# Mixing weights that travel with the token numbers, and a new order for the last two experts' loads

## The reference

```python
# 1: attention inside 16 clusters (q, k, v: 2 x 8 x 768 x 64); x has shape (1536, 512)
# 2: mixture of 8 experts, each takes exactly cap = N // 8 = 192 tokens
order = np.argsort(-(x @ w_gate).flatten())
for idx in order:
    tok, e = (int(idx) // E, int(idx) % E)
    if assigned[tok] >= 0 or counts[e] >= cap:
        continue
    assigned[tok] = e
    counts[e] += 1
for e in range(E):
    mask = assigned == e
    out[mask] = np.maximum(x[mask] @ w1[e], 0.0) @ w2[e]
# 3: 4 dense experts, mixed by given weights
p = domain_probs / (domain_probs.sum(-1, keepdims=True) + 1e-09)
for e in range(4):
    out += p[:, e:e + 1] * (np.maximum(x @ v1[e], 0.0) @ v2[e])
```

## Time and profile before

| | us |
|---|---|
| median of 3 runs (lowest, highest) | 1040.72 (1040.03, 1041.43) |
| the profiled execution | 1038.46 |
| its span in the trace | 1036.7 |
| PE busy | 1002.0 (97%) |
| DVE, ACT, POOL busy | 605.8, 444.0, 440.9 |

### The profile page before, as it was taken

How to read it: one execution, slowest core, us unless ns; L and a number is a source line. 1 busy time by engine, 2 the same in 40 slices (tenths; PEclk the granted TensorE clock), 3 DMA queues, 4 the chain that set the end, 5 groups by cost and what they waited for, 6 DMA issues and landing times.

```text
span 1036.7 us, 18055 instructions
## 1 busy us (share of the span) xinstructions
PE 1002.0 (97%) x6542; PEld 920.8 (89%) x6542; DVE 605.8 (58%) x1320; ACT 444.0 (43%) x862; POOL 440.9 (43%) x360
## 2 busy tenths in 40 slices
PE   5999999999998999998999999999999999999996
PEld 4889999999987999998998899998899998899995
DVE  4888888888866444444224555544487544455542
ACT  4888888888830111111333233223253323233320
POOL 5042323233101111112575875565557765576542
PEclk9999999999999999999999999999999999999998
DMA  4223232323155967679921221221212421221201
GB/s 113 74 77 85 76 83 80 80 82 78 30 124 116 228 167 153 206 190 239 210 60 63 79 65 62 82 72 51 83 41 82 142 81 43 82 75 50 80 1 62
DMA packets 87745, 99.62 MB, mean 96 GB/s; under 512 B 18560, under 2 KB 57472, under 8 KB 87680
## 3 DMA queue, kind: packets, MB, share of 16 engines
q1 hardware_dynamic: 84976, 92.40, 33.0%
q0 software_dynamic: 2704, 6.33, 2.0%
HBM read 79.81 MB, written 6.32 MB: 83 GB/s over the span
## 4 chain that ended last, share of the span: by engine, by line
PE 92%; DVE 3%; ACT 2%; DMA 1%; POOL 1%; issue 1%; SPq 0%; DVEq 0%; POOLq 0%
PE ps_y L1431 9%; PE ps_y L1432 9%; PE ps_y L1430 9%; PE ps_h L1457 9%; PE ps_y L1472 7%; PE ps_h L1432 6%; PE ps_h L1430 6%; PE ps_h L1431 6%; PE ps_t L1335 6%; PE ps_s L1322 4%; PE ps_s L1323 3%; PE ps_o L1350 3%; PE ps_o L1349 3%; PE ps_m L1296 2%; PE ps_m L1369 2%; PE ps_m L1282 1%
## 5 line engine op out<-in xcount | busy, mean ns | idle before, releaser
L577 POOL TENSOR_TENSOR w_lo<-w_sum,w_hi 128x1792 fp32r<-128x1792 f32 x32 | 129.8, 4078 | 62.4 <-ACT w_hi L795 62.4
L1432 PE MATMUL ps_y<-b_lo,h_hi 128*128 128x512 f32 x384 | 149.7, 390 | 0.0
L1431 PE MATMUL ps_y<-b_hi,h_lo 128*128 128x512 f32 x384 | 149.7, 390 | 0.0
L1430 PE MATMUL ps_y<-b_hi,h_hi 128*128 128x512 f32 x384 | 149.4, 389 | 0.0
L1249 DVE SCALAR_TENSOR_TENSOR Y<-ps_y,mix_n,Y 128x512 f32<-128x512 f32 x84 | 63.0, 750 | 134.9 <-PE ps_y L1432 134.9
L1430 PE MATMUL ps_h<-x_hi,w_hi 128*128 128x384 f32 x384 | 128.6, 335 | 0.0
L1432 PE MATMUL ps_h<-x_lo,w_hi 128*128 128x384 f32 x384 | 128.5, 335 | 0.0
L1431 PE MATMUL ps_h<-x_hi,w_lo 128*128 128x384 f32 x384 | 128.4, 334 | 0.0
L583 POOL TENSOR_TENSOR b_lo<-b_raw,b_hi 128x2048 fp32r<-128x2048 f32 x16 | 74.0, 4626 | 115.2 <-ACT b_hi L802 115.2
L974 DVE TENSOR_TENSOR p_lo<-ps_t,p_hi 128x384 fp32r<-128x384 f32 x192 | 100.0, 548 | 27.9 <-ACT p_hi L725 26.3
L965 DVE TENSOR_REDUCE neg_max<-ps_s 128x1 f32<-128x768 f32 x96 | 91.3, 951 | 17.9 <-PE ps_s L1323 17.9
(11 more groups left out here) (203 smaller groups left out, 2224.8 us busy)
## 6 DMA issues: line engine op xcount, KB each, us to landing
w_sum<-in_moe_w_dram SPq DMA_DIRECT2D x64, 256.0 KB, 3.2
b_raw<-in_moe_w_dram SPq DMA_DIRECT2D x16, 1024.0 KB, 5.2
raw_a<-in_moe_w_dram SPq DMA_DIRECT2D x8, 1024.0 KB, 8.7
raw_b<-in_moe_w_dram SPq DMA_DIRECT2D x8, 1024.0 KB, 13.0
odd_a<-in_moe_w_dram SPq DMA_DIRECT2D x8, 1024.0 KB, 7.5
odd_b<-in_moe_w_dram SPq DMA_DIRECT2D x8, 1024.0 KB, 14.7
khhT<-kqT SPq DMA_DIRECT2D x32, 192.0 KB, 2.8
raw_k<-in_k_dram SPq DMA_DIRECT2D x16, 192.0 KB, 2.4
```

What stands on the lines that cost most here:

```text
L577: g.tensor_tensor(w_lo[t][:], w_sum[t][:, 1:8], w_hi[t][:].bitcast(F32), ALU.subtract).then_inc(wlo_done[t], 1)
L1430: t_.matmul(dst, w_hi, x_hi, start=first, stop=False)
L1431: t_.matmul(dst, w_lo, x_hi, start=False, stop=False)
L1432: return t_.matmul(dst, w_hi, x_lo, start=False, stop=last)
```

## The change

`place` gets 12 more columns per tile: each of the four mixing weights in three bf16 parts whose sum is the fp32 number (DVE splits them at the start, four more instructions after L1029; `domain_probs` is loaded in the layout of `place`). The one-hot product then has 14 columns instead of 2 and yields token number and weights; a new function `token_mix(n)` adds the three parts (three DVE instructions on 96 x 8 elements) and leaves the four weights behind the token number in `ids`, 5 words per slot. `keep_ids` waits for it and stores 192 pieces of 20 bytes instead of 192 of 4 bytes. One load brings all 1536 slots' 5 words back to `ids_all`; the 12 gathers, the second read of the numbers and the store of `mix_rows` are gone. Stage 3 takes its factors from `ids_all`. In the last part of the search `token_ids(6)` is written ahead of `take_slots(7)`. On SP the w2 loads of expert 6 wait for its row gather as those of the others do, and the w1 loads of expert 7 wait until both halves of w2 of expert 6 have landed.

```diff
@@ SP, expert_weights(n)
                 to_a, to_b = (((raw_a, a_in), (raw_b, b_in)), ((odd_a, odd_a_in), (odd_b, odd_b_in)))[n % 2]
+                if n == E - 1:
+                    sp.wait_ge(b_in[1], 16 * (n // 2 + 1))
                 for i in range(2):
                     at_least(sp, h_full, 8 * (n - 2) + 4 * i + 4)
                     load_a(*to_a, 0, e, i)
                 at_least(sp, y_full, 2 * (n - 2) + 2)
-                if n < E - 2:
+                if n < E - 1:
                     sp.wait_ge(gathered, 32 * (n + 1))
@@ POOL
             def keep_ids(n):
                 first = n * CAP
-                g.dma_start(ids_dram[first:first + CAP].rearrange("(s p) o -> p (s o)", s=2), ids[0:CAP // 2, n, :],
-                            allow_slow_non_contiguous=True).then_inc(ids_out[n >= EARLY], 16)
+                pool.wait_ge(mix_ready, n + 1)
+                g.dma_start(ids_dram[first:first + CAP].rearrange("(s p) o -> p s o", s=2), ids[0:CAP // 2, n],
+                            allow_slow_non_contiguous=True).then_inc(ids_out, 16)
...
-            for n in range(EARLY):
+            for n in range(E):
                 expert_rows(n)
                 keep_ids(n)
-            pool.wait_ge(ids_out[0], 16 * EARLY)
-            ids_by_tile(0, 0, T_EARLY)
...
-            for t in range(T_EARLY, NT):
-                mix_rows(t)
+            pool.wait_ge(ids_out, 16 * E)
+            g.dma_start(ids_all[:], ids_dram.rearrange("(t p) o -> p t o", p=P),
+                        allow_slow_non_contiguous=True).then_inc(ids_back, 16)
@@ DVE, at the start
+            mlink(v_.tensor_copy(place[:, :, 2:2 + E2], mix_n[:]), 5)
+            mlink(v_.tensor_tensor(mix[:], mix_n[:], place[:, :, 2:2 + E2], ALU.subtract), 6)
+            mlink(v_.tensor_copy(place[:, :, 2 + E2:2 + 2 * E2], mix[:]), 7)
+            mlink(v_.tensor_tensor(place[:, :, 2 + 2 * E2:], mix[:], place[:, :, 2 + E2:2 + 2 * E2],
+                                   ALU.subtract), 8)
@@ DVE, search
+            def token_mix(n):
+                HS = CAP // 2
+                at = ps_tok[0:HS, 0:2 * W].rearrange("p (s a) -> p s a", s=2)
+                link(v_.tensor_copy(mix_lo[0:HS], at[:, :, 2 + 2 * E2:]))
+                link(v_.tensor_tensor(mix_mid[0:HS], mix_lo[0:HS], at[:, :, 2 + E2:2 + 2 * E2], ALU.add))
+                v_.tensor_tensor(ids[0:HS, n, :, 1:].bitcast(F32), mix_mid[0:HS], at[:, :, 2:2 + E2],
+                                 ALU.add).then_inc(mix_ready, 1)
...
                         link(v_.tensor_tensor(dig[:], dig_i[:, 1:ND, :], unit[:], ALU.mult))
+                        if n > 0:
+                            token_mix(n - 1)
                     dve.wait_ge(cnt_full, ND * n + i + 1)
...
+            token_ids(E - 2)
+            token_mix(E - 2)
             take_slots(E - 1)
-            token_ids(E - 2)
             slots_hot(E - 1)
             token_ids(E - 1)
+            token_mix(E - 1)
@@ PE, slot_tokens(n)
                 pe.wait_ge(hot_ready, n + 1)
-                at_least(pe, ids_ready, n)
+                pe.wait_ge(mix_step, 8)
+                at_least(pe, mix_ready, n)
...
-                        mm = t_.matmul(ps_tok[:, 2 * s:2 * s + 2], slot_hot[:, c:c + P],
+                        mm = t_.matmul(ps_tok[:, W * s:W * s + W], slot_hot[:, c:c + P],
                                        place[:, t, :], start=(t == 0), stop=(t == NT - 1))
@@ DVE, stage 3
-            dve.wait_ge(mix_in, 16 * NT)
+            dve.wait_ge(ids_back, 16)
```

More of the change, by code:

```diff
@@ L72, in clustered_attention_two_moes @@
     x_dram = nc.dram_tensor("x_rows", (N, DM), F32, kind="Internal").ap()
-    mix_dram = nc.dram_tensor("mix_rows", (N, E2), F32, kind="Internal").ap()
-    ids_dram = nc.dram_tensor("slot_token", (N, 1), I32, kind="Internal").ap()
+    ids_dram = nc.dram_tensor("slot_token", (N, 1 + E2), I32, kind="Internal").ap()
     with ExitStack() as ctx:
@@ L99, in clustered_attention_two_moes @@
         first_c = sb("first_c", [P, C], F32)
-        place = sb("place", [P, NT, 2], BF16)
+        place = sb("place", [P, NT, 2 + 3 * E2], BF16)
         place_f = sb("place_f", [P, NT, 2], F32)
@@ L203, in clustered_attention_two_moes @@
         place_lo = sb("place_lo", [P, 2], F32)
-        ids = sb("ids", [P, E, 2], I32)
+        ids = sb("ids", [P, E, 2, 1 + E2], I32)
+        mix_lo = sb("mix_lo", [P, 2, E2], F32)
+        mix_mid = sb("mix_mid", [P, 2, E2], F32)
         e_num = sb("e_num", [P, E], I32)
-        ids_all = sb("ids_all", [P, NT], I32)
+        ids_all = sb("ids_all", [P, NT, 1 + E2], I32)
         mix = sb("mix", [P, NT, E2], F32)
@@ L281, in clustered_attention_two_moes @@
         gathered = sem("gathered")
-        ids_out = [sem(f"ids_out{i}") for i in range(2)]
-        ids_back = [sem(f"ids_back{i}") for i in range(2)]
+        ids_out = sem("ids_out")
+        ids_back = sem("ids_back")
+        mix_ready = sem("mix_ready")
         probs_in = sem("probs_in")
-        mix_in = sem("mix_in")
         mix_step = sem("mix_step")
-        mix_stored = sem("mix_stored")
         a_in = [sem(f"a_in{i}") for i in range(2)]
@@ L485, in _ @@
             pool.wait_ge(const_ready, 9)
-            g.tensor_copy(place[:], place_f[:]).then_inc(const_ready, 1)
+            g.tensor_copy(place[:, :, 0:2], place_f[:]).then_inc(const_ready, 1)
             def search_constants():
@@ L589, in rows_out @@
                     t = out_tile(gr, q)
-                    g.indirect_dma_start(out, bass.IndirectOffsetOnAxis(ap=ids_all[:, t:t + 1], axis=0),
+                    g.indirect_dma_start(out, bass.IndirectOffsetOnAxis(ap=ids_all[:, t, 0:1], axis=0),
                                          Y[:, t, :], None).then_inc(out_done, 16)
@@ L598, in expert_rows @@
                     g.indirect_dma_start(rows_in[0:CAP // 2, s, :], None, x_dram,
-                                         bass.IndirectOffsetOnAxis(ap=ids[0:CAP // 2, n, s:s + 1], axis=0)
+                                         bass.IndirectOffsetOnAxis(ap=ids[0:CAP // 2, n, s, 0:1], axis=0)
                                          ).then_inc(gathered, 16)
@@ L1086, in slots_hot @@
                                  spread(slot[:, n % 2], 2, hot), ALU.is_equal).then_inc(hot_ready, 1)
+            W = 2 + 3 * E2
             def token_ids(n):
@@ L1245, in outputs @@
                     if J % (2 * E2) == 0:
-                        v_.tensor_scalar(Y[:, t, :], o_ps[q % 3], mix_n[:, t, ex:ex + 1], None,
+                        v_.tensor_scalar(Y[:, t, :], o_ps[q % 3], ids_all[:, t, 1 + ex:2 + ex].bitcast(F32), None,
                                          ALU.mult).then_inc(o_taken, 1)
                     else:
-                        v_.scalar_tensor_tensor(out=Y[:, t, :], in0=o_ps[q % 3], scalar=mix_n[:, t, ex:ex + 1],
+                        v_.scalar_tensor_tensor(out=Y[:, t, :], in0=o_ps[q % 3], scalar=ids_all[:, t, 1 + ex:2 + ex].bitcast(F32),
                                                 in1=Y[:, t, :], op0=ALU.mult, op1=ALU.add).then_inc(o_taken, 1)
-            dve.wait_ge(mix_in, 16 * NT)
+            dve.wait_ge(ids_back, 16)
             for J in range(NJ):
@@ L1622, in _ @@
             pe.wait_ge(h_taken, 8 * E)
-            pe.wait_ge(ids_ready, E)
+            pe.wait_ge(mix_ready, E)
             pe.wait_ge(slot_ready, E)
```

31 lines of the change are left out of this document (5 added, 26 removed).

## The result

The changed kernel takes 1033.18 us (median of 4 runs, 1032.57 to 1034.64), the kernel before 1040.65 beside it: ratio 0.993, 95% interval 0.9916 to 0.9944, 7.5 us less. In two later groups (a group is a set of kernels run in turn on one chip, each time with the kernel before beside them) the ratio of the two was 0.9929 (0.9906 to 0.9951) and 0.9952 (0.9935 to 0.9968). The profiled executions differ by less than the medians: 1038.46 and 1032.57, 5.9 us.

A forecast was written before the change was run, and what follows sets the result against it. The prediction took PE, busy 97% of the span, as the bound, with expert 6's late gather as what could pay: -3.22 (stall) - 1.80 (clock) + 0 = -5.0 us, median 1040.72 to 1035.7, own range 1034.5 to 1037.2, 8-in-10 range 1034.5 to 1042.0.

The forecast's parts named there:

- Steps 1 and 2: At expert 6: PE's stall for gathered rows goes, 3.22 us, and the slow clock after it, 1.80 us; together 5.02.
- step 1: Expert 6's token numbers ready 2.6 us earlier on DVE, gather lands in 3.1 us, PE not held up; gain 3.22 us.
- rival (c): Expert 6's gather still lands 6.3 us after issue, stall 0.6 us instead of 3.2: 1038.1 us; chance 0.08.
- Step 3: DVE's added work, token_mix at 0.57 us per expert and four instructions at the start, is hidden; cost taken as 0.
- Step 4: PE's one-hot products widen from 2 to 14 columns; upper bound 0.5 us, cost taken as 0.
- Step 5: POOL loses 13 DMAs, some 13 us, before the handover to stage 3; hidden, gain 0, stage 3's span unchanged.
- Step 6: Expert 6's w2 loads, issued later, still land in time if the new 20-byte store takes up to 5 us; cost 0.
- (a): Store lasts as now, so the wait moves to expert 6's w2, 2.5 us late (0 to 6): 1040.0 us; chance 0.26.
- (b): Store lasts longer than now, so w2 of experts 3 and 6 comes late: 2.6 us slower, 1043.3 us; chance 0.10.
- the second rival: Another name for (b): the store of token numbers lasts longer than now, 1043.3 us; chance 0.10.

The follow-up runs named there:

- the 20-byte run: Kernel before with both orders changed (DVE and loads), 12 gathers kept, its 4-byte token-number pieces put 20 bytes apart in DRAM: 1035.07 us, ratio 0.9918 to the kernel before.

## Why the prediction was right, and where it fell short

**Steps 1 and 2, the stall and the clock:** right, to 0.0 us in the profiled executions (3.22 + 1.80 forecast, 5.02 measured), and the transposes run without idle time. Inside step 1 one reading was off. The second gather took 4.7 us from issue to landing and not 3.1, as w1 of expert 6 was not through by 477: 404 GB/s still moved from 477 to 478. Expert 5's 3.1 us, which rival (c) read as taken under the same load, were not: that gather was issued at 451.68, and the load beside it ended sooner (211 GB/s from 452 to 453). It did no harm, since the gather was issued at 476.50 and PE came at 483.30, which left room for 6.8. What step 1 put down to the order on DVE alone was shared: in the changed kernel the held-back `raw_b` does it as well.

**Step 3:** right as far as the runs can tell. `token_mix` takes 0.16 us an instruction and is hidden in the phases. In phase 1 PE waits for DVE's `full_k`, in the first profile for 0.53 us, and the stall behind it is shorter (1.75 us and not 2.37). How much of that wait is `token_mix` is open: of eleven profiles without it eight have the same wait with 0.9 us and three have none, and of seven with it in its first place three have 0.5 and four 0.8 to 0.9.

**Step 4:** right. In the chain, 24 products with 14 columns take 0.59 us, with 2 columns 0.58.

**Step 5:** right for this kernel, wrong as it was argued. With the dense store and the stall gone, the chain over the gathers does come onto the path (3.8 us in that profile). The forecast asked only when PE needs the low parts; what was late was ACT's `h`, which stands behind `w_hi` in ACT's queue. With the store spread out and all 12 gathers kept it is hidden; in the changed kernel it is also 12 DMAs shorter.

**Step 6:** right, and for the reason that was given. For expert 3 the store lands in 2.7 us instead of 9.9 and w2 in 6.7 instead of 13 to 16; nothing is late. Its reason, the spacing, is the one that the 20-byte run shows. Rivals (a) and (b) both needed a long store; (a) is what the kernel with both orders and the dense store does. Against the rows stood two rules of the Trainium skill ("DMA: Bandwidth & Descriptors"): taking turns packet by packet (section on queues, rings and completion order), and the read-modify-write below 512 bytes (Specifications). The measurement decides against both as a forecast of this case. By the first, `raw_b` would have been in time whatever the store does; with the dense store it was 5.73 us late. By the second, 20 bytes would cost what 4 do, which is rival (a) and not, as the prediction says there, the second rival; for expert 3, 4 bytes 20 apart took 2.7 us to land, as 20 bytes did. Two stores of 192 pieces of 4 bytes, which both rules treat alike, differed by a factor of 3 in landing and by 9.5 us in the kernel's time. Whether a read-modify-write is at work in them no run shows.

**The step that failed is the one from the profile to the median:** "I take the difference that the sum gives and apply it to the median". The stall was sized at 5.0 us from one execution, while in five it cost 4.9 to 8.9, on average 6.1. The median of before lay 2.3 us above its profile, which was the hint: this wait, beside loads, differed from one execution to the next (3.22 to 4.21 us), and with it went much of the spread. The kernel before spread over 7.8 to 9.4 us in three groups, the changed kernel over 2.6 in one of them. In the last group both spread little and alike (4.1 and 4.6 us), and there the difference of the medians was 5.3 us, near the sum. The changed kernel's median lies 0.6 above its profile. In numbers: 5.0 in the stretch, 0.2 ahead of it and 0.6 at the end make 5.9 between the profiles; the other 1.6 of the 7.5 is what the median of before loses over its profile and the changed kernel does not. Of the latter the profiles show 1.1 (6.1 against 5.0); the rest is not explained and would lie in executions that were not profiled. The 0.6 at the end is a term that the fifth step put at nothing ("the span of stage 3 is PE's own"). The mechanism of the sum was right; its size was that of one cheap execution.

## What to carry to other kernels

A tiny store can cost the transfers beside it far more than itself: look at what the other queues move while it lands, and try its pieces spread over DRAM when loads are moved to stand beside it. That alone need not pay: here the spacing gained nothing while the stall was there. A wait that is removed uncovers the next one on the same path; here both a late w2 and a chain over POOL and ACT stood right behind it. The order on DVE alone gained 3.5 us, both orders with the dense store nothing, and the whole gain came with the spread store and either order. Where the median lies well above the profiled run, size a stall from several profiles, and reckon that its removal can give back the scatter too.

## What the runs showed of the hardware that was not expected

- 192 stores of 4 bytes side by side in DRAM landed in 8.3 to 10.0 us (medians of a profile; expert 7's took 19.4 us in one) and held loads on another queue to 9 GB/s; the same 192, 20 bytes apart, in 2.6 to 2.8, and the changed kernel's loads moved at 368 GB/s in the same window (that kernel's pieces are 20 bytes long and back to back). Whether the spacing has to be 20 bytes, or which part of the memory path is at work, was not tried.
- The time from the last output's issue to the end of the span fell from 7.3 to 6.2 us with the gathers gone, at 0.5 us more outside the span; three more semaphores do not change it.
- The same stall left the granted clock at its lower level for 3.4 us of the 8 from 488 to 496 in one execution (0.57 and 1.00) and for 5.8 us in another (0.50 and 0.77).
